# Attention weights turned by VectorE in 32x32 blocks, value products in eight array tiles

## The reference, cut to what matters

```python
# q, k, v: (4 batches, 8 heads, 576 rows, 64)
scores = q @ k.T / 8 + bias[head]            # bias: small MLP (1 -> 32 -> 8) of log1p|i-j| / log1p(i)
attn   = exp(scores - rowmax); attn /= rowsum + 1e-9
x      = attn @ v                            # -> (2304 tokens, 8*64 = 512)
x      = top-1 mixture of 8 experts(x)       # 512 -> 1024 -> 512, gated
out    = maximum of three products(x) @ w_out
```

## Time and profile before

| | |
|---|---|
| median of 3 runs | 1023.03 us |
| profiled execution, own time | 1019.65 us |
| its span, first to last instruction | 1017.9 us |
| mean granted clock of PE | 0.988 |
| bias stage | 0 to about 62 us |
| attention | to 355.5 us |
| routing, experts, last layer | from 356.4 us |

### The profile page before, as it was taken

How to read it: one execution, slowest core, us unless ns; L and a number is a source line. 1 busy time by engine, 2 the same in 40 slices (tenths; PEclk the granted TensorE clock), 3 DMA queues, 4 the chain that set the end, 5 groups by cost and what they waited for, 6 DMA issues and landing times.

```text
span 1017.9 us, 19575 instructions
## 1 busy us (share of the span) xinstructions
PE 960.7 (94%) x6722; PEld 796.5 (78%) x6722; DVE 526.8 (52%) x1071; ACT 385.4 (38%) x807; POOL 285.5 (28%) x310
## 2 busy tenths in 40 slices
PE   6889999999999866999999999999999999999998
PEld 3466776767767565788888888888999999999997
DVE  7976676666756458444444466445433333333331
ACT  6887777777777470332000033034211111111100
POOL 6204501001010037976200078177620101010100
PEclk9999999999999987999999999999999999999999
DMA  5765544444443167764200056156211010100001
GB/s 156 269 203 148 151 112 104 117 111 115 108 96 98 46 219 233 233 206 129 90 21 21 22 167 209 41 163 192 99 63 32 32 32 32 32 30 3 26 6 31
DMA packets 125752, 106.79 MB, mean 105 GB/s; under 512 B 88072, under 2 KB 91304, under 8 KB 125688
## 3 DMA queue, kind: packets, MB, share of 16 engines
q1 hardware_dynamic: 86408, 56.26, 19.0%
q10 hardware_dynamic: 33824, 34.03, 11.6%
q0 software_dynamic: 5456, 15.60, 4.8%
HBM read 78.94 MB, written 26.90 MB: 104 GB/s over the span
## 4 chain that ended last, share of the span: by engine, by line
PE 58%; POOL 5%; issue 1%; DVE 1%; ACT 0%; ACTq 0%; POOLq 0%
PE moe_banks L1673 22%; PE moe_banks L1628 12%; PE moe_banks L1594 12%; PE moe_banks L1690 7%; POOL slots L1362 3%; PE moe_banks L1612 2%; PE moe_banks L1531 1%; POOL x_behind L1372 1%; PE moe_banks L1579 1%; POOL x_tok L1372 1%; PE moe_banks L1656 1%; PE moe_banks L1540 0%; POOL x_tok L1400 0%; DVE in_lane L1775 0%; ACT slots L1470 0%
## 5 line engine op out<-in xcount | busy, mean ns | idle before, releaser
L1673 PE MATMUL moe_banks<-yT,slots 128*128 128x384 f32 x1080 | 193.2, 334 | 0.0
L1673 PEld LDWEIGHTS moe_banks<-yT,slots 128*128 128x128 f32 x1080 | 187.9, 188 | 0.6
L1362 POOL TENSOR_TENSOR slots<-x_tok,slots 128x512 fp32r<-128x512 f32 (+1 forms) x116 | 141.1, 1252 | 155.7 <-ACT slots L1470 155.2
L1470 ACT CAST slots<-x_tok 128x512 fp32r<-128x512 f32 (+1 forms) x116 | 67.9, 602 | 258.8 <-PE moe_banks L1594 127.8
L1594 PE MATMUL moe_banks<-slots,xT 128*128 x600 | 146.4, 400 | 4.3 <-ACT slots L1470 3.1
L1628 PE MATMUL moe_banks<-slots,hT 128*128 x600 | 140.3, 389 | 0.8 <-POOL slots L1362 0.8
L779 DVE CUSTOM_DVE_ANT_0 probs<-s_ps,bias 128x576 f32<-128x576 f32 x144 | 103.7, 753 | 67.0 <-PE s_ps L627 48.2
L1594 PEld LDWEIGHTS moe_banks<-slots,xT 128*128 128x128 f32 x600 | 113.0, 192 | 28.8 <-issue 5.4
L1628 PEld LDWEIGHTS moe_banks<-slots,hT 128*128 128x128 f32 x600 | 112.6, 188 | 24.3 <-issue 1.0
L889 ACT ACTIVATE probs<-probs,negmax 128x576 f32<-128x576 f32 x144 | 110.6, 770 | 14.9 <-DVE negmax L779 14.5
L1928 DVE TENSOR_TENSOR best<-best,moe_banks 128x384 f32<-128x384 f32 x36 | 19.9, 553 | 132.0 <-PE moe_banks L1673 127.6
(11 more groups left out here) (207 smaller groups left out, 1187.9 us busy)
## 6 DMA issues: line engine op xcount, KB each, us to landing
x_tok<-in_moe_w ACTq DMA_DIRECT2D x96, 256.0 KB, 3.0
bias_table<-staged SPq DMA_DIRECT2D x36, 296.0 KB, 3.3
bias<-bias_table SPq DMA_DIRECT2D x32, 288.0 KB, 2.7
result_rows<-y SPq DMA_DIRECT2D x25, 256.0 KB, 3.2
x_tok<-in_moe_w ACTq DMA_DIRECT2D x24, 192.0 KB, 2.4
k_raw<-in_k SPq DMA_DIRECT2D x32, 128.0 KB, 2.4
q_raw<-in_q SPq DMA_DIRECT2D x32, 128.0 KB, 2.5
v_raw<-in_v SPq DMA_DIRECT2D x32, 128.0 KB, 2.3
```

The costliest lines, as they stand in the source:

```text
L1362: nc.gpsimd.tensor_tensor(rest, raw(n, rows), near.bitcast(F32), ALU.subtract).then_inc(part_done(e, part)[0], 1)
L1470: nc.scalar.copy(near, raw(n, rows)).then_inc(near_done, 1)
L1673: last = nc.tensor.matmul(u_ps[m], final_weight(far, slots, m, d, a, f), yT[:, c, d, :], start=(d == 0 and k == 0), stop=(d == KD - 1 and ...
```

## The change

Three inputs are laid out anew before the launch (`lay_out`): queries and keys with the 64 dimensions of both batches of a pair on the 128 partitions, the queries' last 64 rows of each batch with zeros in the other's place; values in 18 blocks of 32 keys. The transposes of keys, queries and weights on PE go, with their copies out.

```diff
+            def turn(it, u, s):                       # VectorE
+                ...
+                for b in range(2 if s < COMB else 1):
+                    dve.wait_ge(exped, ...)
+                    nc.vector.transpose(pT[u][:, turned_tile(s, b), :],
+                        probs[:, step, b * SEQ:(b + 1) * SEQ]).then_inc(turned, 1)
```

```diff
+        VALUES = {0: range(0, 6), 1: range(6, 12), 2: range(12, KEY_BLOCKS)}     # KEY_BLOCKS = 18
             def values(it, u, blocks):
                 if blocks[0] == 0:
+                    pe.wait_ge(turned, TILES * n + TILES)
+                    pe.wait_ge(v_in[u], 16 * it + 16)
+                    pe.wait_ge(x_copied, n)            # from the second unit on
+                for c in blocks:
+                    for a in range(QUADRANTS):         # 4
+                        lanes = slice(a * HIDDEN, (a + 1) * HIDDEN)
+                        for b in range(2):
+                            shared = b == a // 2
+                            ...                        # 5 tiles of 32 columns if shared, else 4
+                            last = nc.tensor.matmul(o_ps[b * DH:(b + 1) * DH, a, columns],
+                                v_raw[u][lanes, b, c, :], pT[u][lanes, tiles, c * HIDDEN:(c + 1) * HIDDEN], ...)
```

```diff
+            def head(it, first, last):                # VectorE, in every step
+                add_bias(*after(it, u, s)); if s == 0: invert(*previous)
+                turn(it, u, s)
+                if s == COMB and not last: query_rests(it + 1, u)
+            # ScalarE, in every step
+                exponentials(*after(it, u, s))
+                if s >= COMB - 1 and not last:
+                    (key_nears, query_nears)[s - (COMB - 1)](it + 1, u)
+                if s == COMB - 1: store_output(*previous)
+                if s == COMB: copy_output(*previous)
+            # GpSimd
+            def key_rests(it, u): ...                 # kT rest = k_raw - near, 128x576
+            def scale_outputs(it, u): ...             # x_tok rows *= inv, 128x576
```

In the bias stage the load of `both` moves from SP's to ACT's queue, VectorE no longer waits for the loads of `w2`, and its two small copies to `base` move behind step 1:

```diff
-    LOADS = 16 * (3 + G)
+    LOADS, W2_LOADS = 16 * 3, 16 * G
-        dve.wait_ge(const_mm, 1)
-        nc.vector.tensor_copy(base[0:LAST, :], first_bank[...])      # now after step RING - 2
```

More of the change, by code:

```diff
@@ L288, in build_attention @@
         o_filled, o_emptied = sem("o_filled"), sem("o_emptied")
-        inv_eps = sem("inv_eps")
-        inv_done = sem("inv_done")
+        inv_eps, inv_done = sem("inv_eps"), sem("inv_done")
+        x_filled, x_copied, x_scaled = sem("x_filled"), sem("x_copied"), sem("x_scaled")
         STEPS = COMB + 1
[L294 to L303, removed]
@@ L371, in build_attention, with prepared @@
         SCALE = 1.0 / float(np.sqrt(DH))
[L373 to L378, removed]
-        def store_rows(eng, it, u):
[L382 to L388, removed]
+        def prepared(it, u, first, last):
+            return None if last else (it + 1, u)
+        def store_rows(eng, it, u):
+            eng.wait_ge(x_scaled, unit(it, u) + 1)
             eng.dma_start(x_dram.rearrange("(t p) d -> p t d", p=P)[:, u * TILES:(u + 1) * TILES, bass.ds(it * DH, DH)],
@@ L711, in head, with outputs @@
+                if blocks[-1] == KEY_BLOCKS - 1:
+                    last.then_inc(o_filled, 1)
+            def outputs(it, u):
+                pe.wait_ge(o_emptied, unit(it, u) + 1)
+                for tile in range(FULL + 1):
+                    to = x_ps[0][:, tile * P:(tile + 1) * P] if tile < FULL else x_ps[1]
+                    last = nc.tensor.transpose(to, out_T[:, tile * P:(tile + 1) * P], ident[:])
+                last.then_inc(x_filled, 1)
             def head(it, first, last):
@@ new lines, in copy_output @@
+            def copy_output(it, u):
+                act.wait_ge(x_filled, unit(it, u) + 1)
+                head = bass.ds(it * DH, DH)
+                for b in range(2):
+                    first = u * TILES + b * (COMB + 1)
+                    nc.scalar.copy(x_tok[:, first:first + FULL, head],
+                                   x_ps[0].rearrange("p (t b d) -> p t b d", b=2, d=DH)[:, :, b, :])
+                for b in range(2):
+                    part = slice(b * REM, (b + 1) * REM)
+                    last = nc.scalar.copy(x_tok[part, u * TILES + COMB, head], x_ps[1][part, b * DH:(b + 1) * DH])
+                last.then_inc(x_copied, 1)
@@ L954, in _ @@
             heads_loop(act, head)
-            for group in range(GROUPS):
-                store_output(HEADS - 1, 1, group)
+            store_output(HEADS - 1, 1)
+            copy_output(HEADS - 1, 1)
 EXPERTS = 8
```

505 lines of the change are left out of this document (167 added, 338 removed).

## The result

| | before | after |
|---|---|---|
| median of 4 runs each | 1024.24 us (1022.48 to 1025.49) | 1085.37 us (1081.54 to 1093.51) |
| ratio | | 1.061 (1.054 to 1.067) |
| profiled execution: own time, span | 1019.65, 1017.9 us | 1093.51, 1091.7 us |
| mean granted clock | 0.988 | 0.90 |

The account below looks back on a forecast made before the run. PE, busy 94% of the span, was taken as the bound in attention. 15 x (18.0 - 15.3) = 40.5, plus 1.9, less 0.8, gave 41.6 us: 1023.03 to about 982 us; likeliest case 965 to 1001, 8-in-10 range up to 1015.

Parts of the forecast that it names:

- DMA: Value loads: 0.29 MB a unit grow to 1.18, needing 188 GB/s; fits, since the bias stage runs at 256.
- zero, give or take 1.5 us: Bias stage: cost of adding two unit value loads while the small key and query rows go.
- the 1.9 of the forecast: Start: gain of 0.7 us from loads and copies off the path plus 1.2 us of DVE work in the bias stage.
- rival 3: Attention: the clock falls as PE is less busy; unit 21 us, 1065 us; chance 0.14 together with the half-rate DVE transposes.
- rival 2: DVE transposes at half rate, 1.28 instead of 0.68 us each; about 1050 us; chance 0.14 together with the falling clock.
- rival 1: Value products on PE: records start no faster than 26 ns, values 7.5 instead of 4.9 us, 1020 us; chance 0.07.
- The stall for the query nears: Step 4 of each unit: DVE's query_rests waits for ACT's query_nears, idling DVE 0.9 us a unit.
- The unit of 15.3 us: Each attention unit: 15.3 us against 18.0, with DVE's work and waits setting its length.
- the sum of the forecast: Unit length: DVE work 13.4, stall 0.9, 0.4 more if store_output is late, ten handovers 0.6; 15.3 us.
- All 15 intervals: Attention, unit to unit: each was to shrink from 18.0 to 15.3 us, 40.5 us in all.
- The end: Last unit, without cover, up to the routing: 14.0 us against 13.2, a loss of 0.8 us.
- the 982: Whole kernel: forecast median of about 982 us from 1023.03, with 978 for the profiled execution; likeliest case's chance 0.68.

Follow-up runs that it names:

- e1: Kernel after, a unit's values loaded by four DMAs, one per quadrant, instead of one with four copies outermost: ratio to before 1.0041, median 1030.5 us.
- e9: e6 with head 0's value loads moved out of the bias stage, and head 2's bias tiles loaded ahead of its weights: ratio to before 0.989, 1012.4 us.
- e4: Kernel before plus an unneeded copy of the same extra bytes per unit, as four DMAs of 32 rows each: ratio to before 1.0052, 1030.3 us.
- e3: Kernel before plus one unneeded copy at each value load, its four copies outermost: ratio to before 1.074, 1101.1 us.
- e5: e1 with ScalarE's order of output copies, query and key nears changed in a unit's last two steps: ratio to before 1.0055, 1025.3 us.
- e6: e1 plus two groups of four unused matmuls per unit in PE's idle times: ratio to before 0.9984, 1018.1 us.
- e8: e1 with e5's ScalarE order, e6's unused matmuls, and head 0's value loads behind the bias stage: ratio to before 0.9990, 1018.0 us.
- e10: e9 with ScalarE's order changed as in e5: ratio to before 0.986, 1008.9 us.
- e11: e10 with VectorE's query_rests ahead of the comb step's transpose instead of behind it: ratio to before 0.985, 1009.3 us.
- e13: e11 with TensorE's loop over heads 1 to 6 written out, other engines unchanged: ratio to before 1.023, 1043.4 us.
- e12: e11 with half of the unused matmuls, two groups of two per unit: ratio to before 0.978, 1003.6 us.

## Why the prediction was wrong, step by step

**The step that failed** is DMA: "188 GB/s. The bias stage runs at 256, so it fits", and for the two loads in the bias stage "zero, give or take 1.5 us". It compared bytes a second of the whole path, and never asked how many engines one transfer uses. In the wide form the same bytes do fit: e1 moves 168 and e9 184 GB/s from 130 to 300 us, and e4 pays 0.5%. In the form of the change, on four engines by the packets in flight, they cost 58 us in this kernel (after against e1), and a like transfer cost 76 in the kernel before (e3). No row of before could show it, since the earlier trace rows are of other loads, but the form stood in the diff, and it needed a rival of its own. Of the bias stage's +26 us, 21 to 25 go with the form (88.7 to 67.4, 65.6 and 64.1 in e1, e5 and e6); 7 to 10 more go when the loads leave the stage (57.5), which makes it 5 us shorter than before, against the 1.9 of the forecast. So even in the wide form two loads in that stage are not "zero".

**The clock** was rival 3, but taken as all or nothing (a unit of 21 us, 1065 us) and small. It is neither. Once the form is right the clock falls in every unit for part of it, 17.1 against 15.3 us (e1 and e6). The argument "in the bias stage, busy 83%, 1.00" didn't carry over to a kernel in which PE is idle for 1.09 and 1.25 us at one place of every unit (e1).

**Right in mechanism and size.** Transposes on DVE take 755 ns, two in 1.43, so 0.68 apart: rival 2 is out. Six blocks of values take 1.91 us with the last record's 0.27, 1.64 against 1.65: rival 1 is out, for 96 records here start 17 ns apart in eight tiles. The 25 ns between starts that the Trainium skill gives (TensorE: Matmul & The Clock Gate, "Wait — 56ns, not 53.3ns?") don't hold across these tiles; the measurement decides. The stall for the query nears is 1.0 us a unit (0.9 forecast), though it turned out not to be on the path. The unit of 15.3 us came out to the tenth in the looped units of e6, e8, e9, e10 and e11, but that is luck in part: these kernels run eight unused matmuls a unit that the forecast didn't have, and since e10 and e11 took DVE's stall away and the unit stayed, it isn't the sum of the forecast (13.4 of DVE + 0.9 + 0.4 + 0.6) that sets it. From 200 to 292 us, six units, DVE is busy for 82.8 us in e6 and 89.5 in e10.

**Wrong in size.** All 15 intervals were priced alike. e13 shows that the first run of the code makes a unit long by itself. Of the first interval some 6 us go with the place of the value loads: it takes 17.7 us in e6, which loads them in the bias stage, and 23.4 in e9, which loads them behind it and has the stage 7 us shorter. How much of the rest is code, and how much GpSimd's work and other loads, was not separated. The end, by the measure of the first table, was to take 14.9 us and takes 19.5 to 22.2 in the versions in eight tiles: the values 9.0 us in e6 in place of 5.2, for the most part, and the rest behind them.

**What is left of the 982.** e11's profiled execution took 1009.4 us against the 978 that the sum gave for one, 31.4 more. Its stages: the bias stage to unit 0's comb scores -4.2 (66.6 against 70.8); the looped units 0; the first three and the last two intervals 8.3 + 3.9 + 4.1 + 1.7 + 6.5 = 24.5, rounding and the rest of the units 0.9; the end 20.9 - 14.9 = 6.0; routing and experts 4.1. That is 31.3. The last follows neither the form nor attention's clock, but it goes with the chip: where the kernel before took 1019.1 and 1020.1 us in the median (e5 to e8, e13), this part took 660.5 to 663.3 us, and where it took 1024.2 to 1025.1 (e1 to e4, e9 to e12), 662.6 to 666.1. Since no kernel was profiled on two chips this is likely and not shown.

## What to carry to other kernels

For each transfer that a change adds or reshapes, ask how many DMA engines its outermost dimension lets it use, before adding up bytes: a transfer on few engines holds up everybody's packets while the page shows a half idle DMA. When PE stops being the full engine, look for the places where it will be idle (here 1.1 and 1.25 us a unit), price the stretch behind them at half clock as a case of its own, and price first passes of code in small tiles by themselves. A wait that goes is a gain only if the engine is on the path: try the next engine in the chain before counting it.

## What was not expected of the hardware

- A 1.18 MB load with four copies outermost: 15.3 us, four packets at a time. As four DMAs: 5.7 to 7 us, 16 at a time, though each packet of 9216 bytes takes 0.68 instead of 0.36 us.
- Plain float32 records of 32x64 tiles, eight tiles in turn: 96 in 1.64 us, 17 ns from start to start.
- Unused matmuls made the program faster (e6, 7 us less than e5 on the same chip), and half as many faster again (e12, 6 us less than e11 on the same chip, intervals touching).
- PE code in straight line comes at 256 instructions in 4.0 us (e6's last values); a loop's later rounds don't pay it.
- DVE's query_rests beside a POOL operation: 1.79 us instead of 0.82. `invert`'s first instruction rises in e11, from 0.24 (e6) to 0.81 us in the mean, while the 128x576 transposes stay at 0.756.
